# Input chunks transposed by VectorE in 32x32 blocks and sent through a DRAM scratch, in place of transposes on TensorE

## The reference, cut to what matters

```python
# attention: 2 x 4096 tokens, 192 channels in 8 heads of 24; 7 taps backwards in time
w = softmax over the 7 taps of weight_gen[b, s, head, :]
att[b, s, head, :] = sum over k of w[k] * x_padded[b, s + k, head, :]
x = att.reshape(8192, 192)
h = x @ moe_w_in                    # 192 x 2048
x = (h * cos(h)) @ moe_w_out        # 2048 x 192
h = x @ moe2_w_in
out = max(0.01 * h, h) @ moe2_w_out # float32 throughout
```

## Time and profile before

| | |
|---|---|
| median of 3 runs | 1157.13 us (1156.3 to 1157.22) |
| profiled execution, its own time | 1155.77 us |
| its span in the profile | 1153.6 us |
| TensorE busy | 1137.1 us, 99% of the span |
| VectorE busy | 917.8 us, 80% |
| ScalarE busy | 724.0 us, 63% |
| mean granted TensorE clock | 0.999 |

### The profile page before, as it was taken

How to read it: one execution, slowest core, us unless ns; L and a number is a source line. 1 busy time by engine, 2 the same in 40 slices (tenths; PEclk the granted TensorE clock), 3 DMA queues, 4 the chain that set the end, 5 groups by cost and what they waited for, 6 DMA issues and landing times.

```text
span 1153.6 us, 23282 instructions
## 1 busy us (share of the span) xinstructions
PE 1137.1 (99%) x9990; PEld 939.9 (81%) x9990; DVE 917.8 (80%) x897; ACT 724.0 (63%) x774; POOL 86.0 (7%) x80
## 2 busy tenths in 40 slices
PE   7899999999999999999999999999999999999998
PEld 5778888888888888888888888888888888888876
DVE  8998898878889788797887869878797787978433
ACT  6666674766657676574755757566575655757553
POOL 5860000000000000000000000000000000000000
PEclk9999999999999999999999999999999999999999
DMA  9670100101001010100101001010100101000001
GB/s 262 196 129 1 35 2 11 40 1 50 1 15 36 1 49 1 49 1 8 43 1 49 1 13 38 1 49 2 38 13 4 46 1 49 1 9 7 1 15 28
DMA packets 70334, 37.41 MB, mean 32 GB/s; under 512 B 56796, under 2 KB 66394, under 8 KB 69848
## 3 DMA queue, kind: packets, MB, share of 16 engines
q1 hardware_dynamic: 65784, 30.68, 10.3%
q0 software_dynamic: 4448, 5.24, 2.6%
HBM read 29.61 MB, written 6.29 MB: 31 GB/s over the span
## 4 chain that ended last, share of the span: by engine, by line
PE 94%; DVE 1%; issue 0%; ACT 0%; ACTq 0%
PE slot L1124 44%; PE acc_a L1124 29%; PE acc_b L1124 19%; DVE g_lo L870 0%; PE slot L1056 0%; PE acc_b L1097 0%; PE slot L1060 0%; PE acc_a L1090 0%; DVE gate L951 0%; PE acc_b L1098 0%; PE acc_a L1089 0%; PE acc_a L1088 0%; DVE gate L977 0%; DVE prods L377 0%; DVE fold L891 0%
## 5 line engine op out<-in xcount | busy, mean ns | idle before, releaser
L1124 PE MATMUL acc_a<-g_hi,out_hi_lo 64*128 64x512 f32 x2000 | 696.6, 388 | 0.0
L870 DVE TENSOR_TENSOR g_lo<-gate,g_hi 128x1024 fp32r<-128x1024 f32 x252 | 310.6, 1233 | 111.7 <-ACT g_hi L683 111.1
L1124 PEld LDWEIGHTS acc_a<-g_hi,out_hi_lo 64*128 64x128 f32 x2000 | 367.8, 184 | 37.4 <-issue 0.5
L1124 PE MATMUL acc_b<-g_hi,out_hi_lo 64*128 64x512 f32 x1000 | 388.5, 389 | 4.3 <-DVE g_lo L870 2.8
L1124 PE MATMUL acc_b<-g_lo,out_hi_lo 64*128 64x512 f32 x1000 | 386.6, 387 | 0.0
L1124 PE MATMUL acc_a<-g_lo,out_hi_lo 64*128 64x512 f32 x1000 | 386.6, 387 | 0.0
L683 ACT ACTIVATE g_hi<-gate 128x1024 fp32r<-128x1024 f32 x252 | 267.1, 1060 | 103.5 <-PE acc_b L1124 81.8
L1124 PE MATMUL slot<-x_a_hi,in_a_lo 64*128 64x512 f32 x1024 | 298.1, 391 | 1.8 <-DVE g_lo L870 1.4
L1124 PE MATMUL slot<-x_b,in_b_hi 64*128 64x512 f32 x1024 | 296.0, 387 | 0.2 <-DVE x_b L884 0.2
L1124 PE MATMUL slot<-x_a_lo,in_a_hi 64*128 64x512 f32 x1024 | 295.8, 387 | 0.0
L1124 PE MATMUL slot<-x_a_hi,in_a_hi 64*128 64x512 f32 x1024 | 295.7, 386 | 0.0
(11 more groups left out here) (104 smaller groups left out, 1032.0 us busy)
## 6 DMA issues: line engine op xcount, KB each, us to landing
x_win<-in_x SPq DMA_DIRECT2D x14, 960.0 KB, 4.8
out<-turned_a SPq DMA_DIRECT2D x240, 16.0 KB, 1.5
out<-turned_b SPq DMA_DIRECT2D x120, 16.0 KB, 1.5
out_raw<-in_moe_w_out SPq DMA_DIRECT2D x3, 512.0 KB, 8.4
out_hi_lo<-in_moe_w_out POOLq DMA_DIRECT2D x2, 768.0 KB, 10.8
out_hi_lo<-in_moe_w_out POOLq DMA_DIRECT2D x1, 1536.0 KB, 14.2
taps_w<-in_weight_gen SPq DMA_DIRECT2D x2, 560.0 KB, 9.4
in_a_raw<-in_moe_w_in SPq DMA_DIRECT2D x1, 1024.0 KB, 5.2
```

Of the source, the lines that this page charges most:

```text
L870: nc.vector.tensor_tensor(g_lo[:, q % 2, :], result_of(i - b, q), g_hi[:, q % 2, :].bitcast(FP32), ALU.subtract)\
L1124: return nc.tensor.matmul(to, w[rows, :], x[rows, :], start=start, stop=stop)
```

## The change

From chunk 2 on, TensorE no longer transposes the input. After the last add, VectorE transposes `prods[:, 0, :]` in 32x32 blocks into `prods[:, 1, :]` (`turn_input`). SyncE then issues four stores of 32 partitions each from `prods[:, 1, :]` to a scratch in DRAM (`x_columns`, 192 x 512, two of them by turns), waits until all four have landed, and issues two loads, 128 and 64 partitions by 512 elements, into `x_raw_a` and into part of `result`. ScalarE and VectorE split from these two SBUF tiles, at step 16 of their program order instead of 15. The order of the tokens in a chunk changes with it, so chunks 0 and 1, which TensorE still transposes, are written to the slot in the new order, the result is copied out of PSUM without the reordering that it had, and the stores read 32-element pieces of `turned_a` and `turned_b` with a stride.

```diff
+    x_columns = nc.dram_tensor("x_columns", (2, dim, N), FP32, kind="Internal").ap()
...
+            def move_input(c):
+                columns = x_columns[c % 2]
+                sp.wait_ge(x_turned, c - 1)
+                for k in range(P // BLOCK):
+                    sp.dma_start(columns[:, k * P:(k + 1) * P].rearrange("(n d) t -> d n t", d=BLOCK),
+                                 prods[k * BLOCK:(k + 1) * BLOCK, 1, :].rearrange("d (n t) -> d n t", t=P))\
+                        .then_inc(x_put, 16)
+                sp.wait_ge(x_put, PUTS * (c - 1))
+                if c > 2:
+                    sp.wait_ge(x1_ready, 2 * c)
+                sp.dma_start(x_raw_a[:, :], columns[0:DA, :]).then_inc(x_moved, 16)
+                sp.dma_start(x_raw_b, columns[DA:dim, :]).then_inc(x_moved, 16)
...
+            move_input(2)
             load_x(3)
-            store(0)
-            load_x(4)
-            for i in range(3, C - 2):
+            for i in range(2, C - 1):
+                move_input(i + 1)
                 store(i - 2)
-                load_x(i + 2)
-            for c in range(C - 4, C - 1):
+                if i + 2 < C:
+                    load_x(i + 2)
+            for c in range(C - 3, C - 1):
                 store(c)
...
             def split_high(i, step, chunk):
-                act.wait_ge(filled, fills(i, step))
...
+                if chunk >= 2:
+                    act.wait_ge(x_moved, MOVES * (chunk - 1))
+                    nc.scalar.activation(x1_a_hi[:, :], x_raw_a[:, :], ACT.Copy).then_inc(x1_hi, 1)
+                    nc.scalar.activation(x1_b[0:DB, :], x_raw_b, ACT.Copy).then_inc(x1_hi, 1)
...
-                if step == INPUT_STEP - 1 and input_splits(i, INPUT_STEP):
+                if step == INPUT_STEP and input_splits(i, INPUT_STEP):
                     split_high(i, INPUT_STEP, i + 1)
...
+            def turn_input(c):
+                dve.wait_ge(att, (c + 1) * ATT_STEPS)
+                nc.vector.transpose(prods[:, 1, :],
+                                    prods[:, 0, :].rearrange("p (j d r) -> p d j r", j=J, r=BLOCK))\
+                    .then_inc(x_turned, 1)
...
-                if step == INPUT_STEP - 1 and input_splits(i, INPUT_STEP):
+                if step == INPUT_STEP and input_splits(i, INPUT_STEP):
                     split_low(INPUT_STEP, i + 1)
...
                         todo.pop(0)()
+                        if not todo:
+                            turn_input(i + 1)
...
-            def rest_of_iteration(i, q):
-                after = UNITS[q] + 1
-                if after == INPUT_STEP and kind(i, after) == "input":
-                    both_products(i, q, i, q - LAG, lambda: wait_for_input(i, INPUT_STEP))
-                    transpose_input(slots[INPUT_STEP % SLOTS])
-                else:
-                    both_products(i, q, i, q - LAG)
```

More of the change, by code:

```diff
@@ L78, in window_attention_two_ffn @@
     gen_rows = weight_gen.rearrange("b (p t) h k -> (b p) (t h) k", t=per_part)
+    x_columns = nc.dram_tensor("x_columns", (2, dim, N), FP32, kind="Internal").ap()
     out_rows = out.rearrange("(p t) d -> p (t d)", t=per_part)
     def kind(i, step):
-        if step == (FIRST_INPUT_STEP if i == 0 else INPUT_STEP):
-            return "input" if i <= C - 2 else None
+        if i == 0 and step == FIRST_INPUT_STEP:
+            return "input"
         if step in FIRST_UNITS:
@@ L94, in input_splits @@
             return step == FIRST_INPUT_SPLIT
-        return kind(i, step) == "input"
+        return step == INPUT_STEP and i <= C - 2
     def first_out(i, step):
@@ L207, in window_attention_two_ffn @@
         result = sb("result", [P, J, dim])
+        x_raw_a = sb("x_raw_a", [P, N])
         turned_a = sb("turned_a", [P, N])
@@ L269, in window_attention_two_ffn @@
         turned = sem("turned")
+        x_turned = sem("x_turned")
+        x_put = sem("x_put")
+        x_moved = sem("x_moved")
         result_ready = sem("result_ready")
@@ L332, in wait_for_chunk @@
                     engine.wait_ge(att, done)
-                    engine.wait_ge(filled, fills(c - 2, INPUT_STEP) if c > 1 else 1)
+                    if c <= 2:
+                        engine.wait_ge(filled, fills(0, INPUT_STEP) if c == 2 else 1)
+                    else:
+                        engine.wait_ge(x_put, PUTS * (c - 2))
             def wait_for_halo():
@@ L459, in result_of, with of_blocks @@
             return gate[:, q % 2, :]
+        PUTS, MOVES = 16 * P // BLOCK, 16 * 2
+        x_raw_b = result[:, :, :].rearrange("p t d -> p (t d)")[0:DB, 0:N]
+        def of_blocks(t):
+            return t.rearrange("p (k j t) -> p k j t", j=J, t=BLOCK)
         STORES = J * dim // BLOCK
@@ L537, in store @@
                         sp.dma_start(to[:, j, :, DA + d:DA + d + BLOCK],
-                                     turned_b[s:s + BLOCK, j % 2 * P:(j % 2 + 1) * P]
-                                     .rearrange("t (k d) -> t k d", d=BLOCK)).then_inc(stored, 16)
+                                     turned_b[s:s + BLOCK, :]
+                                     .rearrange("t (k j d) -> t k j d", j=2, d=BLOCK)[:, :, j % 2, :])\
+                            .then_inc(stored, 16)
             def store_last():
@@ L691, in split_high @@
             def split_high(i, step, chunk):
-                act.wait_ge(filled, fills(i, step))
[L694 to L698, removed]
+                if chunk >= 2:
+                    act.wait_ge(x_moved, MOVES * (chunk - 1))
+                    nc.scalar.activation(x1_a_hi[:, :], x_raw_a[:, :], ACT.Copy).then_inc(x1_hi, 1)
+                    nc.scalar.activation(x1_b[0:DB, :], x_raw_b, ACT.Copy).then_inc(x1_hi, 1)
+                else:
+                    act.wait_ge(filled, fills(i, step))
+                    slot = slots[step % SLOTS]
+                    nc.scalar.activation(halves(x1_a_hi[:, :]), slot[:, :, 0:N // 2], ACT.Copy)\
+                        .then_inc(x1_hi, 1)
+                    nc.scalar.activation(halves(x1_b[0:DB, :]), slot[0:DB, :, N // 2:N], ACT.Copy)\
+                        .then_inc(x1_hi, 1)
                 if chunk <= 2:
@@ L710, in leave_res_a @@
                     act.wait_ge(turned, 2 * (i - 1) - 1)
[L712 to L715, removed]
+                to, sums = res_a[:, :], acc_a[:, :]
+                if i == LAST:
+                    to, sums = to.rearrange("p (j k t) -> p k j t", j=J, t=BLOCK), of_blocks(sums)
+                nc.scalar.activation(to, sums, ACT.Copy).then_inc(acc_a_out, 1)
             def move_result(i, step):
@@ L880, in split_low @@
                 dve.wait_ge(x1_hi, chunk * 2 + 2)
+                if chunk >= 2:
+                    nc.vector.tensor_tensor(x1_a_lo[:, :], x_raw_a[:, :], x1_a_hi[:, :].bitcast(FP32),
+                                            ALU.subtract).then_inc(x1_ready, 1)
+                    nc.vector.tensor_tensor(x1_b[DB:P, :], x_raw_b, x1_b[0:DB, :].bitcast(FP32),
+                                            ALU.subtract).then_inc(x1_ready, 1)
+                    return
                 nc.vector.tensor_tensor(halves(x1_a_lo[:, :]), slot[:, :, 0:N // 2],
@@ L901, in leave_res_b @@
                 fold_b(phase)
-                parts = [t.rearrange("p (k h j r) -> p h j k r", k=2, h=2, j=2)
-                         for t in (acc_b[0:DB, :], fold[:, :])]
+                last = phase == second_phase(LAST)
                 for h in range(2):
-                    ins = nc.vector.tensor_tensor(
-                        res_b[h * DB:(h + 1) * DB, :].rearrange("p (j k r) -> p j k r", j=2, k=2),
-                        parts[0][:, h], parts[1][:, h], ALU.add)
-                ins.then_inc(acc_b_out, 1)
+                    to = res_b[h * DB:(h + 1) * DB, :]
+                    to = to.rearrange("p (j k t) -> p k j t", j=2, t=BLOCK) if last else \
+                        to.rearrange("p (k j t) -> p k j t", j=2, t=BLOCK)
+                    parts = [of_blocks(t)[:, :, 2 * h:2 * h + 2, :] for t in (acc_b[0:DB, :], fold[:, :])]
+                    ins = nc.vector.tensor_tensor(to, *parts, ALU.add)
+                ins.then_inc(acc_b_out, 1)
+            def turn_input(c):
[3 more added lines that the diff above has]
+                    .then_inc(x_turned, 1)
             def turn_result(i):
@@ L1051, in transpose_input, with columns @@
             def transpose_input(slot):
+                def columns(t):
+                    return t.rearrange("p (h j t) -> p j h t", j=J, t=BLOCK)
                 for j in range(J):
@@ L1055, in transpose_input @@
                         rows = slice(k * DB, (k + 1) * DB)
-                        nc.tensor.transpose(slot[:, k, j * DB:(j + 1) * DB],
+                        nc.tensor.transpose(columns(slot[:, k, 0:N // 2])[:, j],
                                             prods[rows, 0, j * dim:j * dim + DA], ident[rows, rows])
@@ L1060, in transpose_input @@
                         ins = nc.tensor.transpose(
```

(6 more changed lines are left out.)

10 lines of the change are left out of this document (4 added, 6 removed).

## The result

The changed kernel takes 1206.84 us (median of 4 runs, 1202.29 to 1208.28) against 1157.06 before: a ratio of 1.0425, 95% interval 1.0397 to 1.0453. The forecast was 1186.5, with a range of 1165 to 1212. The mechanism is the one forecast, a wait of TensorE once an iteration; it is larger than forecast, and a second cost came with it.

The account below looks back on a forecast made before the run. TensorE, busy 1137.1 of 1153.6 us, was taken as the bound; later starts of unit 0, 11 x 1.72 + 3 x 3.50 = 29.4 us with the 8.0 gain included, gave 1186.5 us against the median, range 1165 to 1212.

Parts of the forecast that it names:

- My own sign that the prediction would be wrong: Any of: last add over 2 us early against TensorE, both landings together under 3 us, granted clock leaving 1.00.
- The gain of 8.0 us: TensorE's transposes of chunks 2 to 15 removed: 14 x 0.57 = 8.0 us.
- The chain as the cost, and carried once an iteration: Hand-overs from VectorE's last add to unit 0 delay TensorE 1.72 us in 11 iterations, 3.50 in 3.
- My sum to the fourth pair: Steps from last add through transpose, stores, loads, copies and subtractions, summed to 9.55 us counted to unit 0's start.
- the second load's landing: 128 KB load behind the 256 KB one: 2.4 us from its issue, bounds 1.5 and 3.7.
- The time there was: From last add to unit 0's start before the change: 7.83 us ordinarily, 6.05 in iteration 3.
- The clock: Rival: TensorE's waits at unit 0 halve its clock for one unit, 14 x 4.31 = 60 us, about 1247; chance 0.06.
- What I cost at nothing: VectorE's extra 1.01 us, the queue's later stores and window load, ScalarE's later `g_hi`, GpSimd's copy, result copies, strided stores: zero.
- The transfers hidden anyway: Rival: chain takes at most 7.26 us, so the transposes are simply gone, 1149; chance 0.06.
- VectorE as the bound: Rival: transfers hidden, but VectorE's extra transpose costs whole at steps 7 to 12, +6 us, 1163; chance 0.04.
- The shortest landings: Rival: store and load landings both 1.5 us, 1.2 us less an iteration, 1170; chance 0.13.
- The estimate by the Trainium skill: Fixed 2.0 us per transfer plus bytes: landings 2.2 and 2.4 instead of 1.8 and 2.4, 6 us more, about 1192.

Follow-up runs that it names:

- e1: Changed kernel without VectorE's input transpose, the scratch stores and the loads, the split reading a zeroed tile: 1150.64 us, ratio 0.9957 to the kernel before.
- e2: Kernel before, TensorE's transposes kept, with the change's VectorE transpose, stores and loads added and nobody using them: 1159.14 us, ratio 1.0020.
- e5: Changed kernel with the whole attention spread one step earlier (steps 6 to 11): 1157.66 us, ratio 1.0001 to the kernel before.

## Why the prediction was right, and what it mis-sized

- **The number.** The measured 1206.84 lies inside the range, 20.3 us over the forecast, and that is partly luck: the range's upper end was made for slow landings, and about half of what was missing is the clock, which the range left out. My own sign that the prediction would be wrong, a granted clock that leaves 1.00, did appear (0.984 to 0.991). The wait is the mechanism forecast, the clock is not.
- **The gain of 8.0 us.** Right in size for an ordinary iteration (0.55 in e1 against 0.57). Over all it is 5.8 by the medians: I cost the split's later place in VectorE's order at nothing. In iterations 3 and 5 it isn't covered, and they are 0.6 us slower instead of 0.57 faster.
- **The chain as the cost, and carried once an iteration.** Right: e1, e2 and e5 each leave out or cover it, and the loss is gone.
- **Its length.** My sum to the fourth pair was 9.55 + 0.68 - 0.11 = 10.12 us; in iteration 7 it is 10.73, on average of 14 it is 10.83. Link by link: VectorE's transpose 0.98 to 0.99 (forecast 1.01); first store's issue to first load 3.41 (1.56 + 1.8 and a hand-over, 3.40), made of faster issues and a landing of 2.0; first load to first copy 3.35 (0.52 + 2.4 + 0.04 = 2.96); two subtractions 1.70 (1.36). The mis-sized terms are the second load's landing, 2.93 from its issue against 2.4, and the subtraction beside GpSimd, 0.98 against 0.68.
- **The time there was.** I counted from 7.83 and 6.05 us. The average length and these give 37.8 us of loss in place of my 27.9.
- **The clock.** I had it as a rival with 0.06, as if it went one way in all 14 iterations or in none, and at 60 us. It came with the forecast: in 6 of 14, for some 13 us. The row that I set against it shows a time before the first matmul and says nothing of an engine that stops in the middle. The Trainium skill (TensorE: Matmul & The Clock Gate, "Loop structure matters more than you think") had been right to warn of a wait for a transfer between matmuls; the trace agrees, with some 13 us.
- **What I cost at nothing.** VectorE's extra transpose and the traffic: 2.3 us together by e2. ScalarE's and GpSimd's places: nothing of ScalarE's showed; GpSimd's copy showed by its port.
- **The other rivals.** The transfers hidden anyway: not so, the landings together take 5.0 us, not 2.1. VectorE as the bound: e2 speaks against it. The shortest landings: 2.0 and 3.0 instead of 1.5 and 1.5.
- **The estimate by the Trainium skill** (DMA: Bandwidth & Descriptors, "Anatomy of one DMA"). By a fixed 2.0 us and bytes the landings would have been 2.2 and 2.4. The trace has 2.0 for the store, halfway between it and my 1.8; the load took 3.0, more than either.

What stays open: why the second load takes 3 us (stores of 16 KB are queued right behind it in the same queue, and I tried no run without them), whether the packets of instructions cause the late landings, and what makes the clock fall behind one wait and not behind another of the same length.

## What to carry to other kernels

Work taken from the engine that bounds the kernel is paid back only if its replacement is early enough: add up the hand-overs from the producer's last instruction to the consumer's first, every issue and landing in series, and set this against the time that passes there now. A chain that is late by one or two microseconds is best cured by starting it one step sooner, which here was worth 49 us for one changed list and made the change cost nothing, while shortening its links brought 5 to 16. Only both together beat the kernel before, by 3.7 us. When the bounding engine is made to stop, price the clock too: it can cost a third of what the wait costs.

## What the runs showed of the hardware that wasn't expected

- TensorE's granted clock fell to the lower level in or behind a unit 0 whose first wait was 0.97 to 3.59 us long, with up to two shorter waits behind it, in 6 of 14 iterations; behind other waits of the same kind, as ahead of 506 us, it stayed up.
- Two loads of 256 and 128 KB out of DRAM were ready no earlier when they were issued at the same time from two queues (3.47 us from the first issue to ScalarE's first copy) than 0.39 us apart from one (3.35).
- A 64x512 subtraction with both operands in SBUF takes 0.98 us beside a GpSimd copy that is already under way, and 0.69 alone; a 128x512 one that started just before the copy kept its 0.69. The copy took 1.13 us, and 0.62 beside a subtraction with one operand in PSUM.
- Landings of the stores and loads that were over 0.4 us late (46 of 924) all had a 16 KB packet of instructions under way during them; without one, none of 745 was late.
